# Attention and two expert layers on one core: where the two halves of the second layer's output are added, for the first two batches

## The reference

```python
scores = cap * tanh((q @ k.T / sqrt(D)) / cap)
x  = softmax(scores) @ v                 # transposed to (B*S, 768) = (1792, 768)
h  = max(x @ w1, x @ w2, x @ w3)         # 768 x 768 each
x2 = h @ moe_w_out                       # 768 x 768
g, val = x2 @ w_gate, x2 @ w_val         # 768 x 1536 each
out = (g * sigmoid(g) * val) @ moe2_w_out   # 1536 x 768
```

## Time and profile before

| | |
|---|---|
| median of 3 runs | 1079.63 us (1076.57 to 1082.3) |
| the profiled execution | 1078.85 us |
| its span, first to last instruction | 1077.1 us |
| PE busy | 1015.7 us (94%) |
| DVE, ACT, POOL busy | 730.6, 558.4, 616.4 us |
| mean granted TensorE clock | 0.982 of full |
| DMA, mean over the span | 157 GB/s |

### The profile page before, as it was taken

One profiled execution on the slowest core, in us unless ns is written; L12 is line 12 of the kernel. 1 busy time (PEld: TensorE's weight loads), 2 busy tenths in 40 slices (PEclk: granted clock), 3 DMA queues, 4 the chain that ended last, 5 costly groups with the idle time before them and its releaser, 6 DMA issues. The chain is left out here.

```text
span 1077.1 us, 14096 instructions
## 1 busy us (share of the span) xinstructions
PE 1015.7 (94%) x4740; PEld 830.4 (77%) x4740; DVE 730.6 (68%) x956; ACT 558.4 (52%) x936; POOL 616.4 (57%) x562
## 2 busy tenths in 40 slices
PE   7999998796999988999999978999999999999998
PEld 4555554354999977998999967899987899899987
DVE  4788789495567467886348869565658688437864
ACT  6888885792344354544434543443435545444532
POOL 5455547476666554764656645564746666555643
PEclk9999999798999999999999999999999999999999
DMA  7989984944433332432643367333323333453336
GB/s 223 311 291 327 323 284 157 329 146 158 132 110 109 105 95 67 132 107 78 197 142 110 109 205 253 101 109 111 105 86 104 96 109 106 144 166 107 110 120 211
DMA packets 120791, 169.24 MB, mean 157 GB/s; under 512 B 10128, under 2 KB 117648, under 8 KB 120720
## 3 DMA queue, kind: packets, MB, share of 16 engines
q1 hardware_dynamic: 120720, 168.34, 49.8%
HBM read 130.94 MB, written 37.36 MB: 156 GB/s over the span
## 5 line engine op out<-in xcount | busy, mean ns | idle before, releaser
L461 POOL TENSOR_TENSOR w_lo<-whole,w_hi 128x384 fp32r<-128x384 f32 x420 | 473.8, 1145 | 333.2 <-ACT w_hi L588 332.1
L588 ACT ACTIVATE w_hi<-whole 128x384 fp32r<-128x384 f32 x420 | 215.1, 519 | 233.1 <-DMA whole<-s_store 139.0
L538 PE MATMUL acc<-a_hi,w_hi 128*128 128x448 f32 x882 | 325.3, 369 | 8.9 <-POOL w_lo L461 7.6
L538 PE MATMUL acc<-a_lo,w_hi 128*128 128x448 f32 x882 | 322.7, 366 | 0.0
L538 PE MATMUL acc<-a_hi,w_lo 128*128 128x448 f32 x882 | 322.6, 366 | 0.0
L538 PEld LDWEIGHTS acc<-a_hi,w_hi 128*128 128x128 f32 x882 | 166.1, 188 | 29.8 <-issue 8.3
L538 PEld LDWEIGHTS acc<-a_hi,w_lo 128*128 128x128 f32 x882 | 166.1, 188 | 13.2
L538 PEld LDWEIGHTS acc<-a_lo,w_hi 128*128 128x128 f32 x882 | 166.1, 188 | 12.8
L490 PE MATMUL acc<-prob,v_one 112*128 112x448 f32 x384 | 163.3, 570 | 5.8 <-DMA v_one<-v_in 5.8
L538 PE MATMUL acc<-b_hi,w_hi 128*128 128x448 f32 x378 | 142.8, 378 | 23.1 <-POOL w_lo L461 10.6
L538 PE MATMUL acc<-b_hi,w_lo 128*128 128x448 f32 x378 | 139.6, 369 | 0.0
(11 more groups left out here) (61 smaller groups left out, 984.9 us busy)
## 6 DMA issues: line engine op xcount, KB each, us to landing
whole<-s_store SPq DMA_DIRECT2D x240, 192.0 KB, 2.3
whole<-w_in SPq DMA_DIRECT2D x180, 192.0 KB, 2.4
raw_w<-w_in SPq DMA_DIRECT2D x30, 768.0 KB, 8.1
s_store<-sum_w SPq DMA_DIRECT2D x30, 768.0 KB, 6.0
qk_raw<-qk_in SPq DMA_DIRECT2D x24, 448.0 KB, 5.2
v_one<-v_in SPq DMA_DIRECT2D x24, 224.0 KB, 3.8
part_store<-sig SPq DMA_DIRECT2D x24, 224.0 KB, 2.8
sig<-part_store SPq DMA_DIRECT2D x24, 224.0 KB, 3.8
```

The lines of the kernel that those rows point to most:

```text
L461: nc.gpsimd.tensor_tensor(w_lo[:, n % RING, :], whole[:, n % RING, :], w_hi[:, n % RING, :].bitcast(F32), ALU.subtract).then_inc(w_lo_done, 1)
L538: last = nc.tensor.matmul(bank(q, BANK_OF[i]), w[:, n % RING, cols], m[:, i, c, :], start=(i < 4 and c == 0 and t == 0), stop=(c == KCH - ...
L588: nc.scalar.activation(w_hi[:, n % RING, :], whole[:, n % RING, :], ACT.Copy).then_inc(w_hi_done, 1)
```

## The change

For super-batch 0 (`added_in_memory(q)`: `q < 30`) the two halves are no longer added on DVE:

- SP's four stores of a "part" quad (18 to 20) go to the final place in `out`, not to `part_store`.
- In quads 27 to 29 SP's four loads of `part_store`, DVE's four adds and SP's four stores to `out` are gone. C22, C12 and C21 are written by DVE to `sig`, as in a "part" quad; C11 is copied to `sig` by ACT (new, one copy a quad, behind `w_hi` at i = 4).
- POOL issues four transfers a quad that add `sig[:, slot, :]` to the block already in `out` (`accum_op=ALU.add`). They stand in POOL's loop over the weights: slot 3 at i = 5, slot 0 at i = 6, slots 1 and 2 at i = 0 and 1 of the next quad, where i is that of the product n - 8.
- A slot of `sig` is written again only when its addition is complete (`out_added`), on DVE and ACT, where it was `out_stored` ahead of SP's load.

Super-batch 1 (quads 48 to 50, 57 to 59) is as it was; its counts of `part_loaded`, `out_done` and `out_stored` start from zero (`part_index(q) - KCH`).

```diff
+def added_in_memory(q):
+    return q < QUADS
...
+        def out_block(q, slot):
+            kind, g, f = kind_of(q)
+            s = q // QUADS
+            return (out[g, :, 2 * s, :], out[g, :, 2 * s + 1, :], out[g + 3, :, 2 * s, :],
+                    out[g + 3, :, 2 * s + 1, :])[slot]
...
                 if kind == "part":
+                    to = [out_block(q, slot) if added_in_memory(q) else part_store[n, slot, :, :]
+                          for slot in range(4)]
...
-                elif kind == "out":
+                elif kind == "out" and not added_in_memory(q):
...
-                    if kind == "out" and i == 0:
+                    if kind == "out" and not added_in_memory(q) and i == 0:
                         load_part(q, 3)
                         load_part(q, 0)
...
+            def add_slot(q, slot):
+                pool.wait_ge(part_stored[slot], 16 * (part_index(q) + 1))
+                nc.gpsimd.dma_start(out_block(q, slot), sig[:, slot, :],
+                                    accum_op=ALU.add).then_inc(out_added[slot], 16)
+
+            def add_results(q, i):
+                if i == 5:
+                    pool.wait_ge(c22_done, q + 1)
+                    add_slot(q, 3)
+                elif i == 6:
+                    pool.wait_ge(out_copied, part_index(q) + 1)
+                    add_slot(q, 0)
+                elif i == 0 and q > K_OUT21:
+                    pool.wait_ge(c12_done, q)
+                    add_slot(q - 1, 1)
+                elif i == 1 and q > K_OUT21:
+                    pool.wait_ge(c21_done, q)
+                    add_slot(q - 1, 2)
...
+                q, i = divmod(n - AHEAD, PROD)
+                if K_OUT21 <= q < QUADS or q == QUADS and i <= 2:
+                    add_results(q, i)
...
+                elif kind == "out" and added_in_memory(q):
+                    act.wait_ge(prod_done, PROD * q + 5)
+                    if g > 0:
+                        act.wait_ge(out_added[0], 16 * part_index(q))
+                    else:
+                        act.wait_ge(valued, 4 * gv_index(q - 1) + 2)
+                    nc.scalar.activation(sig[:, 0, :], b, ACT.Copy).then_inc(out_copied, 1)
...
             def sig_free(q, slot):
...
+                elif kind == "out" and g > 0:
+                    dve.wait_ge(out_added[slot], 16 * part_index(q))
```

More of the change, by code:

```diff
@@ L221, in build @@
         out_stored = [sem(f"out_stored{i}") for i in range(4)]
+        out_copied = sem("out_copied")
+        out_added = [sem(f"out_added{i}") for i in range(4)]
         x_loaded = [sem(f"x_loaded{i}") for i in range(4)]
@@ L258, in c11_taken @@
                 return part_first, part_index(q) + 1
-            return out_done, 4 * part_index(q) + 2
+            if added_in_memory(q):
+                return out_copied, part_index(q) + 1
+            return out_done, 4 * (part_index(q) - KCH) + 2
         def block_ready(e, slot):
@@ L340, in stores @@
                 if kind == "part":
+                    to = [out_block(q, slot) if added_in_memory(q) else part_store[n, slot, :, :]
+                          for slot in range(4)]
                     if i == 4:
                         sp.wait_ge(c22_done, q + 1)
[L343 removed]
+                        store_slot(to[3], 3, part_stored)
                     elif i == 5:
                         sp.wait_ge(part_first, n + 1)
[L346 removed]
+                        store_slot(to[0], 0, part_stored)
                     elif i == 6:
                         sp.wait_ge(c12_done, q + 1)
[L349 removed]
+                        store_slot(to[1], 1, part_stored)
                         sp.wait_ge(c21_done, q + 1)
[L351 to L352 removed]
+                        store_slot(to[2], 2, part_stored)
+                elif kind == "out" and not added_in_memory(q):
                     if i == 4:
[L354 to L355 removed]
+                        sp.wait_ge(out_done, 4 * (n - KCH) + 1)
+                        store_slot(out_block(q, 3), 3, out_stored)
                     elif i == 5:
[L357 to L358 removed]
+                        sp.wait_ge(out_done, 4 * (n - KCH) + 2)
+                        store_slot(out_block(q, 0), 0, out_stored)
                     elif i == 6:
[L360 to L363, removed]
+                        sp.wait_ge(out_done, 4 * (n - KCH) + 3)
+                        store_slot(out_block(q, 1), 1, out_stored)
+                        sp.wait_ge(out_done, 4 * (n - KCH) + 4)
+                        store_slot(out_block(q, 2), 2, out_stored)
             def load_part(q, slot):
@@ L370, in load_part @@
                 else:
-                    sp.wait_ge(out_stored[slot], 16 * n)
+                    sp.wait_ge(out_stored[slot], 16 * (n - KCH))
                 sp.wait_ge(part_stored[slot], 16 * (n + 1))
@@ L411, in _ @@
                         sp.wait_ge(prod_done, PROD * q + i + 1)
-                    if kind == "out" and i == 0:
+                    if kind == "out" and not added_in_memory(q) and i == 0:
                         load_part(q, 3)
                         load_part(q, 0)
-                    if kind == "out" and i == 1:
+                    if kind == "out" and not added_in_memory(q) and i == 1:
                         load_part(q, 1)
@@ L427, in _ @@
             for i in range(4):
-                sp.wait_ge(out_stored[i], 16 * SUPER * KCH)
+                sp.wait_ge(out_stored[i], 16 * KCH)
+                sp.wait_ge(out_added[i], 16 * KCH)
         @block.gpsimd
@@ L622, in take_c11 @@
                     elif s > 0:
-                        act.wait_ge(out_stored[0], 16 * s * KCH)
+                        act.wait_ge(out_added[0], 16 * KCH)
                     nc.scalar.activation(sig[:, 0, :], b, ACT.Copy).then_inc(max_first, 1)
@@ L789, in add_part @@
                 slot = (3, 0, 1, 2)[n]
-                dve.wait_ge(part_loaded[slot], 16 * (part_index(q) + 1))
+                dve.wait_ge(part_loaded[slot], 16 * (part_index(q) - KCH + 1))
                 nc.vector.tensor_tensor(sig[:, slot, :], operand, sig[:, slot, :],
@@ L799, in sig_free @@
                     dve.wait_ge(part_stored[slot], 16 * part_index(q))
+                elif kind == "out" and g > 0:
+                    dve.wait_ge(out_added[slot], 16 * part_index(q))
+                elif kind == "out":
+                    dve.wait_ge(valued, 4 * (gv_index(q - 1) + 1))
                 elif kind == "max" and g == 0 and n == 0 and s > 0:
-                    dve.wait_ge(out_stored[slot], 16 * s * KCH)
+                    dve.wait_ge(out_added[slot], 16 * KCH)
                 elif kind == "gate" and q % QUADS == K_GV1:
@@ L830, in landing @@
                     return blk[:, result, :]
-                if kind in ("gate", "part") or kind == "max" and third == 0:
+                if kind in ("gate", "part") or kind == "max" and third == 0 or kind == "out" and added_in_memory(q):
                     sig_free(q, slot)
@@ L872, in add_c11 @@
                     dve.wait_ge(max_first, q // QUADS * KCH + g + 1)
-                if kind == "max" and n > 0 or kind in ("val", "out"):
+                if kind == "max" and n > 0 or kind == "val" or kind == "out" and not added_in_memory(q):
                     dve.wait_ge(prod_done, PROD * q + 5)
```

4 lines of the change are left out of this document (2 added, 2 removed).

## The result

| | before | after |
|---|---|---|
| median of 14 runs each, us | 1078.6 (1075.67 to 1082.3) | 1085.01 (1081.44 to 1088.65) |
| profiled execution; its span, us | 1078.85; 1077.1 | 1087.45; 1085.7 |
| PE busy, DVE busy, POOL busy, us | 1015.7, 730.6, 616.4 | 1022.7, 727.6, 621.9 |
| mean granted TensorE clock | 0.982 | 0.974 |

The ratio is 1.0062 (95% 1.0049 to 1.0076): slower by 0.6%. The forecast was 1069, the range ended at 1082.

What follows compares the result with a forecast made beforehand. PE, busy 94%, was taken as the bound, with 14.5 us lost to waits and half speed around quads 27 to 29. Gains of 4.0 + 2.1 + 3.8 = 9.9 us off 1078.85 gave 1069 us; range 1064.5 to 1082.

Steps and rivals of the forecast that it cites:

- DVE's four additions gone: On DVE, 2.8 us a quad removed; the first difference then starts 0.75 us after PE's end in quads 28 and 29.
- E28: The end of PE's last matmul of quad 28, from which later starts and waits are counted; 652.85 us before.
- E29: The end of PE's last matmul of quad 29, from which later starts and waits are counted; 668.89 us before.
- SP's loads gone: In quad 27's full DMA queue, `x_store` loads land 3.0 us earlier, so the first difference no longer waits for them.
- E27: The end of PE's last matmul of quad 27, from which later starts and waits are counted; 635.19 us before.
- Waits for the additions: DVE's C12 and C21 wait for additions; landing taken as 4 us, about 5.1 free, so no cost.
- Rival A: Additions land late, delaying C12 and C21 of quads 28 and 29; slower, 1086 at the upper bound; chance 0.13.
- `w_lo` 218: PE's wait in quad 30: 0.2 us lost, was 2.4 and 1.6 of half speed; gain 3.8.
- Added on POOL: Twelve transfer issues on POOL, taken as 1.1 us each, hidden by POOL's lead over PE; cost nothing.
- The chain behind L742: From DVE's differences, `p1` complete after 4.7 us, `u4` after 8.65, `w_lo` of product 218 after 5.35; these stay.
- Rival C: POOL's issues are dear, above 5 us each, pushing back `w_lo` 218; at 6 us, 1075; chance 0.07.
- Rival B: About half the gain: DMA no emptier in quad 27, or landing 6 to 8 us; 1073 to 1075; chance 0.18.

Runs made afterwards that it cites:

- e8: e1 with slots 1 and 2 of quad 29 issued behind `w_lo` 218 and `u4` of quads 28 and 29 formed directly behind u2; 1074.38 us.
- e1: The change with all four adding transfers of quads 27 to 29 issued at i = 6, ahead of POOL's idle time; 1073.85 us, ratio to before 0.9941.
- e3: The change with its twelve adding transfers replaced by plain stores issued by SP, first half missing in the output; 1073.11 us, ratio to before 0.9939.
- e10a: e3 plus twelve adding transfers of 64 KB from POOL at the change's places, to a tensor nobody reads; 1089.07 us.
- e10b: e3 plus twelve plain transfers of 64 KB from POOL at the change's places, to a tensor nobody reads; 1084.69 us.
- e11: The change with slots 1 and 2 issued together behind `w_lo` 204; 1082.18 us, ratio to before 1.0027.
- e4b: e3 with one more POOL tensor operation ahead of each of `w_lo` 205, 206, 212, 213, 219 and 220; 1073.97 us.
- e2: The change with its twelve POOL transfers as plain stores at the same places, not adding, first half missing; 1075.82 us, ratio to before 0.9973.
- e7_tiny_issues: The kernel before plus twelve plain 128 x 1 transfers (0.5 KB) from POOL at the change's places; 1097.36 us, ratio to before 1.0159.

## Why the prediction was wrong

- **DVE's four additions gone: right.** L790 starts at E28 + 0.95 and E29 + 0.95; forecast 0.75.
- **SP's loads gone: right for the landing, not for its worth.** In quad 27 L790 starts at 639.15, E27 + 0.96 (forecast 0.9). But it stands beside two issues and a `w_lo` and takes 2.23 us, not 0.95. With that `p1` cost 2.3 us, not 0.8.
- **Waits for the additions: right.** 4.9 us to landing against 4 taken and 5.1 free. Rival A did not happen. It was not put hard to the test, since the late `u4` gave the additions more time; in e8, without that wait, a C21 waited 0.69 us for one.
- **`w_lo` 218: right.** Lost 0.4 against 0.2, half speed gone.
- **The failed step** is "*Added on POOL* ... Nothing", with "*The chain behind L742* ... These stay". The length of an issue was taken well (1.1 us; 0.86 to 1.20 measured), and its cover, POOL's lead over PE, held. I asked only what waits for POOL, and not what POOL's row does to DVE beside it. The chain's term of 8.65 us from L742 to `u4` held a pair of 2.8 us; it became 7.07 and 6.16. Lost in all 17.2 us (10.4 + 6.4 + 0.4), not 4.6.
- **Rival C** named the place and the evidence (operations with two inputs in `sig` or `blk` run long beside POOL), but priced it by the issue's own length, at over 5 us each. I gave it 0.07, by a rule on the other direction. The issues were indeed not slowed (0.86 us beside a DVE rest at 646.04, 0.87 beside an idle DVE at 684.49), as the Trainium skill's page "SBUF — State Buffer" (section "Who interferes with whom") has it. The same section says that a DVE instruction with two SBUF inputs contends with a GpSimd instruction that reads SBUF, and that who issues first gets the ports. The trace agrees on the contention (1.16 us a pair alone, 2.0 to 2.8 beside `w_lo`). On who goes first it agrees where no issue is near: in e1 a rest starts at 653.36 and a `w_lo` at 653.37, and the rest takes 0.62 us, the `w_lo` 1.48. Beside an issue it does not: in the change the rest that starts at 646.59, ahead of the `w_lo` at 646.65 but during the issue recorded from 646.04 to 646.91, is the one held for 6.54 us. How an issue changes the contention was the price here.
- **Rival B** had about the right size for a kernel free of the hold: e3 and e1 gain 6 to 7 us, not 9.9, with 1.4 to 2.9 us left for `p1`. Its mechanism, `x_store` still late in quad 27, is there in part in e3 (first difference at E27 + 2.4) and not in e1 (E27 + 0.95), so for e1 the size is luck.

Shown: issues followed by ready `w_lo`, and nothing else tried, bring the hold (e10a, e10b, e11 with, e3, e4b without, e1 moved out). Inferred only, and open: that POOL, with an issue behind it and ready instructions ahead, asks for the shared port again before it has let go of it; the overlapping records (1.57 us at a pace of 0.97) speak for it, though behind a plain issue DVE is held at the same pace without the overlap (1.01 us each).

**The version to keep** is the change with its issues at i = 6, ahead of POOL's idle time (e1): 1073.85 us, 0.6% under before and 1.0 to 1.2% under the change (1073.85/1085.01 = 0.990; by the ratios to before, 0.9941/1.0062 = 0.988).

## What to carry to other kernels

An instruction that is cheap and hidden on its own engine can still cost through what it does to its neighbour: when one is put into a row of work on GpSimd, list VectorE's operations with two SBUF inputs that run beside the row, and who waits for them. Put GpSimd's transfer issues where the engine waits anyway, not among tensor operations that are ready. An adding transfer can take the place of a load, an add and a store; its landing (4.9 to 5.9 us here, 3.4 for a plain store from the same queue) has to be covered.

## What was not expected of the hardware

- The hold itself: pairs of rests of 6 to 8 us, where 1.16 is the time beside an idle POOL and 2.0 to 2.8 beside `w_lo` alone.
- An issue's length goes with its kind, not its bytes: a plain one is recorded for 0.56 us (0.69 at most) at 64 and at 224 KB, an adding one for 0.86 to 1.20 in the change. Adding ones that follow one another closely have longer, overlapping records: up to 1.89 us in e1 (224 KB) and 2.20 in e10a (64 KB).
- An adding transfer takes more of the DMA than its bytes say (packets, MB, share of the 16 engines' time). Twelve of them (2.75 MB) from 628 to 700 us, then the plain ones of e2:

```profile
q0 software_dynamic: 1728, 2.75, 28.6%
```
```profile
q0 software_dynamic: 768, 2.75, 9.8%
```

- Twelve stores of 0.5 KB in 4-byte rows cost 18 us (e7_tiny_issues); why is open.
